# The last Y unit of each batch through DRAM, and another order of work at the tile border

## What is computed

```python
kv  = einsum('bhsd,bhse->bhde', k, v)               # 8 batches, 8 heads, 576 rows, 64 wide
y   = einsum('bhsd,bhde->bhse', q, kv)
y   = y / sqrt(mean(y*y, axis=-1) + 1e-6) * g_norm   # attention output, heads side by side: x
u   = x + ((x^T @ U) @ V)^T                          # rank 32 along the sequence
x2  = u + relu(u @ w_ch1) @ w_ch2                    # 512 -> 2048 -> 512
```

## Time and profile before

| | us |
|---|---|
| median of 3 runs (1273.92 to 1274.13) | 1274.0 |
| the profiled execution | 1274.38 |
| its span | 1272.6 |
| TensorE busy | 1250.0 (98%) |
| VectorE busy | 848.3 (67%) |
| ScalarE busy | 541.1 (43%) |
| GpSimd busy | 103.7 (8%) |

### The profile page before, as it was taken

The page is one execution under the profiler, slowest core; times in us unless marked ns, Lnnn a source line. Parts: engine busy times, 40 slices in busy tenths (PEclk is TensorE's granted clock), DMA queues, the critical chain, the costliest instruction groups (busy, mean ns, idle before and its releaser), DMA issues.

```text
span 1272.6 us, 21543 instructions
## 1 busy us (share of the span) xinstructions
PE 1250.0 (98%) x8248; PEld 1209.0 (95%) x8248; DVE 848.3 (67%) x1227; ACT 541.1 (43%) x859; POOL 103.7 (8%) x108
## 2 busy tenths in 40 slices
PE   7899999999999999999999999999999999999998
PEld 6899999999999999999999999999899898998997
DVE  5886566666656678988898988976543644445344
ACT  4664455554555446554544544543322312223120
POOL 5230000000000000000000000012202102022000
PEclk9999999999999999999999999999999999999999
DMA  9777777778677577473453628272323142240221
GB/s 210 206 188 191 184 189 209 204 188 203 175 208 194 164 246 272 136 252 132 166 177 119 239 91 275 90 202 39 102 65 84 59 102 58 66 120 29 53 59 42
DMA packets 342823, 190.46 MB, mean 150 GB/s; under 512 B 242752, under 2 KB 313296, under 8 KB 342752
## 3 DMA queue, kind: packets, MB, share of 16 engines
q1 hardware_dynamic: 338592, 184.36, 51.3%
q0 software_dynamic: 1600, 4.56, 1.4%
q10 hardware_dynamic: 2560, 0.59, 0.2%
HBM read 115.08 MB, written 72.29 MB: 147 GB/s over the span
## 4 chain that ended last, share of the span: by engine, by line
PE 91%; DVE 4%; issue 2%; DMA 2%; POOL 1%; ACT 1%; ACTq 0%; POOLq 0%; DVEq 0%
PE ps L1532 27%; PE ps L1534 27%; PE ps L1533 27%; PE ps L1553 2%; PE ps L1564 2%; PE ps L1572 1%; DMA w_raw<-in_moe_w_ch 1%; PE ps L1537 1%; DVE x_lo L1160 1%; POOL w_raw L708 1%; PE ps L1820 1%; PE ps L1823 1%; PE ps L1566 0%; PE ps L1590 0%; DVE y_hl L1096 0%
## 5 line engine op out<-in xcount | busy, mean ns | idle before, releaser
L1532 PE MATMUL ps<-x_hi,w 128*128 128x288 f32 x896 | 267.6, 299 | 3.2 <-DVE x_lo L1160 2.5
L1533 PE MATMUL ps<-x_lo,w 128*128 128x288 f32 x896 | 264.3, 295 | 0.0
L1534 PE MATMUL ps<-x_hi,w 128*128 128x288 f32 x896 | 264.0, 295 | 0.0
L1532 PE MATMUL ps<-r_hi,w_hi 128*128 128x384 f32 x672 | 224.8, 334 | 1.0 <-DVE r_lo L1320 1.0
L1533 PE MATMUL ps<-r_lo,w_hi 128*128 128x384 f32 x672 | 224.5, 334 | 0.0
L1534 PE MATMUL ps<-r_hi,w_lo 128*128 128x384 f32 x672 | 224.5, 334 | 0.0
L954 ACT ACTIVATE r_hi<-hb 128x768 fp32r<-128x768 f32 x168 | 142.5, 850 | 166.4 <-PE ps L1534 161.1
L1532 PEld LDWEIGHTS ps<-x_hi,w 128*128 128x128 f32 x896 | 168.1, 188 | 4.8 <-DVE x_lo L1160 3.3
L1534 PEld LDWEIGHTS ps<-x_hi,w 128*128 128x128 f32 x896 | 168.6, 188 | 0.0
L1533 PEld LDWEIGHTS ps<-x_lo,w 128*128 128x128 f32 x896 | 168.4, 188 | 0.0
L1322 DVE TENSOR_TENSOR r_lo<-hb,r_hi 128x768 fp32r<-128x768 f32 x120 | 114.8, 958 | 32.3 <-ACT r_hi L954 32.3
(11 more groups left out here) (168 smaller groups left out, 2332.0 us busy)
## 6 DMA issues: line engine op xcount, KB each, us to landing
hT_scratch<-h_st SPq DMA_DIRECT2D x64, 576.0 KB, 4.2
hb<-hT_scratch SPq DMA_DIRECT2D x24, 1536.0 KB, 7.2
uT_scratch<-x_raw SPq DMA_DIRECT2D x32, 288.0 KB, 3.9
x_st<-uT_scratch SPq DMA_DIRECT2D x24, 384.0 KB, 3.5
x2T_scratch<-x_st SPq DMA_DIRECT2D x24, 384.0 KB, 5.7
x_raw<-x2T_scratch SPq DMA_DIRECT2D x8, 1152.0 KB, 5.7
xt_in<-x2T_scratch SPq DMA_DIRECT2D x144, 64.0 KB, 2.5
k_raw<-in_k SPq DMA_DIRECT2D x64, 128.0 KB, 3.9
```

Source lines behind the costliest of these rows:

```text
L1532: mm(dst, ws[0], xs[0], start=first, stop=False, skip_group_check=chained)
L1533: mm(dst, ws[0], xs[1], start=False, stop=False, skip_group_check=chained)
L1534: return mm(dst, ws[1], xs[0], start=False, stop=last, skip_group_check=chained)
```

## The change

`Y_UNITS` becomes all units from 6 on, so the last unit of each batch (7, 11, up to 31) goes through DRAM too. At the tile border:

- VectorE: sums 2 and 6 and the low half of operand 1 move from steps 52 to 54 to the end of step 55, behind the transposition and addition of the last unit. Sum 4 moves from step 55 to step 1 of the next tile, behind the row sums. The low halves of operands 3 and 4 move from steps 1 and 2 to steps 2 and 4, behind the normalisation and behind the low half of Y. The q transposition of the first unit moves from row 3 to row 6 in every tile (before: in the first tile alone).
- ScalarE: the high half of operand 2 moves from step 53 into the attention copy at step 55, between its two copies. The high halves of operands 3, 4 and 5 move from steps 1, 2, 3 to 2, 3, 4.

```diff
-Y_UNITS = tuple(m for m in range(HP + 2, UNITS) if m % HP < HP - 1)
+Y_UNITS = tuple(range(HP + 2, UNITS))
...
-            def attn_copy(m, bx, by, y=y, units=0):
+            def attn_copy(m, bx, by, y=y, units=0, tile=None):
...
                 nc.scalar.activation(y[:, 0:JM, :].rearrange("p j m -> p (j m)"), ps[:, bx], ACT.Copy).then_inc(s_o, 1)
+                if tile:
+                    x_high(tile[0], tile[1], 2)
                 act.wait_ge(s_out, 2 * m + 2)
...
-            X_HIGH_AT = (27, 34, 53)
-            X_HIGH_THEN = (1, 2, 3, 6)
+            X_HIGH_AT = (27, 34)
+            X_HIGH_THEN = (2, 3, 4, 6)
...
                     elif at_ == ATT and m + 1 < UNITS:
-                        attention_evacuated(m + 1)
+                        attention_evacuated(m + 1, (t + 1, 1 - par) if r == HP - 1 else None)
+                    elif at_ == ATT:
+                        x_high(t + 1, 1 - par, 2)
...
-            X_LOW_THEN = (0, 1, 2, 5, 10)
+            X_LOW_THEN = (0, 2, 4, 5, 10)
...
                     if at_ == 1:
                         sums(m, sq)
+                        if k == 1 and not first:
+                            x_sum(t, par, 4)
...
-                    elif at_ == (6 if first and r == 0 else 3) and m + 1 < UNITS:
+                    elif at_ == (3 if r else 6) and m + 1 < UNITS:
                         q_transposed(m + 1)
...
-                    if k in (33, 53):
-                        x_low(t + 1, 1 - par, (33, 53).index(k))
-                    if k in (52, 54, 55):
-                        x_sum(t + 1, 1 - par, {52: 2, 54: 6, 55: 4}[k])
+                    if k == 33:
+                        x_low(t + 1, 1 - par, 0)
+                    if k == STEPS - 1:
+                        x_sum(t + 1, 1 - par, 2)
+                        x_low(t + 1, 1 - par, 1)
+                        x_sum(t + 1, 1 - par, 6)
...
+                    if k == 1:
+                        x_sum(t, 1, 4)
                     if k in X_LOW_THEN:
                         x_low(t, 1, 2 + X_LOW_THEN.index(k))
```

More of the change, by code:

```diff
@@ L780, in attn_copy, with attention_evacuated @@
                 nc.scalar.activation(y[:, JM, :], bank(by, 0, P), ACT.Copy).then_inc(s_o, 1)
-            def attention_evacuated(m):
-                attn_copy(m, BX, BY, units=min(m + 2, UNITS))
+            def attention_evacuated(m, tile=None):
+                attn_copy(m, BX, BY, units=min(m + 2, UNITS), tile=tile)
                 squares(m, sq)
```

## The result

| | before | after |
|---|---|---|
| median, us | 1273.96 (1273.59 to 1274.13) | 1282.88 (1281.21 to 1283.70) |
| ratio | | 1.0069, 95% interval 1.0051 to 1.0086 |
| profiled execution | 1274.38 | 1282.71 |
| its span | 1272.6 | 1280.9 |

What follows compares the result with a forecast made beforehand. The prediction took TensorE's matmuls to set the pace. Six borders (6.0 us) and the last (1.6) added 7.6 us to the profiled 1274.38: 1282.0, less 0.4 for the median, rounded to 1282; range 1274 to 1287 us.

Steps and rivals of the forecast that it cites:

- The transposes: TensorE, last unit of each batch: five transposes of Y go, 0.55 us saved for each of seven units, 3.9 in all.
- The line behind the arrival: VectorE at the border, from Y's transposition to low half 6: step 12 starts at 173.85 instead of 172.94, +0.9 us.
- break-even: Border: if Y's blocks come back at 159.1 us, freed matmuls pay for the stalls; a tie, 1275 us, chance 0.12.
- full gain: Border: with blocks there by 158.0 us TensorE never waits, each border gives 1.07 us back; 1267 us, chance 0.10.
- The stalls: TensorE at the border waits for late operands, 2.0 us in all, against 1.1 us of gain.
- The arrival: Border: Y's blocks return through DRAM, their transposition on VectorE starting 10.0 us after the normalisation's start, plus 0.1.
- The third rival: Y's DRAM trip by the fit alone: blocks back within some 6 us, kernel faster; counted in the second rival, chance 0.10.
- The moves: Border, VectorE and ScalarE: the later q transposition costs nothing; sum 4's 0.67 us is counted in the VectorE line.
- At most 0.5 us a tile: First unit's q transposition at row 6: upper cost where VectorE's idle 1.6 us no longer covers the later blocks.
- The last border: Behind unit 31: step 6 is 0.3 us late and loads of the second weight add 1.3, together +1.6 us.
- knock-on: Fourth rival: late blocks delay following units, or u's store lands late; 0.5 to 1.4 us a tile more, chance 0.08.
- The sum: Whole kernel: six borders at 0.9 + 0.1 us, 6.0 us, and 1.6 us for the last, +7.6 us.

## Why the prediction was right, step by step

**The transposes.** 0.55 us per unit expected, 0.54 found (a stretch of 14.82 or 14.83 became 14.28), and the low-rank matmuls have no wait. Right.

**The line behind the arrival.** Counted from the transposition, low half 1 was to end 3.1 us later, low half 3 7.5 and low half 6 13.8. The rows of L1164 above give 3.09 (its end at 165.10), 7.48 (169.49) and 13.72 (175.73). Added up from pitches of the earlier trace rows, start to start, it held to a tenth of a microsecond, though VectorE had never run in this order. The break-even was put at 159.1, which is D = 9.1 behind 149.96, and the borders say 9.11; the full gain at 158.0, D = 8.0, and the borders say 7.94.

**The stalls.** Steps 2, 4, 6 and 12 were named and are late. Step 8 and the low-rank part, named too, were not; TensorE had lost time at three steps by then, which is likely why.

**The arrival** is the term that was mis-sized. 10.0 us was taken, with 0.1 added at the end from the queue; 10.49 was measured, and at one to one behind D that is 0.35 us a border, 2.1 us in all. I had put twelve units in one median, and they were of two kinds. The K load stands ahead of Y's store in all of them. In the second units of a batch it is still being issued when Y is finished: the store leaves 1.2 to 1.4 us behind the start of the normalisation, and the trip has a mean of 10.37. In the third it is through by then: the store leaves at 0.86, and the trip has 9.60. The last unit of a batch is of the first kind and a little worse: its store leaves at 1.23 to 2.14, mean 1.53. From the second units alone I would have come within 0.12 us.

**What the trip is made of.** In the mean of the six borders: the normalisation 0.83 us, 0.70 until the store of Y leaves (K's loads stand ahead of it on SP), 3.1 in the middle until a store has landed, 1.3 more until the first block load leaves (V's and q's loads stand ahead), 2.3 for the four block issues, 2.2 until the transposition: 10.5. The Trainium skill, "DMA: Bandwidth & Descriptors", section "Anatomy of one DMA — SWDGE (gpsimd) path", would have a store and a load back within some 6 us of the finished Y (an estimate from its 2.0 us and 436 GB/s, for the other issuing path); the traces have 9.7. Transfer by transfer they don't contradict it: the store lands 3.1 us after its issue in the middle, a block load 2.5. What the estimate has no term for is the 0.7, the 1.3 and the four issues one behind another. The third rival was that sum, and it falls.

**The moves.** Put at nothing, they changed a border by -0.2 us where Y comes early and by +0.1 where it comes late. "At most 0.5 us a tile" for the q transposition was kept: 0.42 in one of six. The run at row 11 showed what lies beyond: five rows later, 26 us.

**The last border.** +1.6 expected, 1.12 found: the step behind the weight's additions starts at 480.55 where before had 470.98, 9.57 us later, and 8.45 of these were there at the last attention (444.75 against 436.30), ahead of unit 31. The loads of the weight came 1.1 us later against VectorE's list (4.57 instead of 3.47) where 1.9 had been counted with. The 0.55 of unit 31's freed transposes, which fall between the last attention and the tile's start, are already off the 1.12.

**What was given back.** From 480.55 on the changed kernel makes up 1.2 us: the rest of the up tile loses 0.35 more, and the down product takes 1.5 us less (349.6 against 351.1, from its first product to its last). Two waits for the low half of its operand (1.0 us in the list before) are not in the list after. The same shows in all nine kernels here in which the last units are no longer transposed on TensorE (349.6 to 350.2 us, against 350.9 to 351.3 in the other three), also where unit 31 is as before. I did not expect it, and its cause stays open.

**The sum and the luck in it.** 8.3 at six borders, 1.1 at the last, 0.4 knock-on, -0.2 in the first tile, -1.2 behind it: 8.4, and the spans differ by 8.3 us. The forecast had 7.6, from 6.0 and 1.6. The sign and the mechanism are as predicted, but that the totals lie only 0.7 apart is partly luck: the borders cost 2.3 us more than forecast, and the last border (0.5) and the down product took most of that off again.

## What to carry to other kernels

A round trip through DRAM is its landings and what is issued ahead of and between them: here some 5.3 us of two landings, 4.3 of issues and queue, and 0.8 of the operation that makes the data. Price it from units of the trace that have the same queue ahead of them, not from all that look alike, and name what its landing gates: the engine's line behind it, summed from start to start, gives a break-even before anything is built. Here 0.54 us of freed matmuls stood against a landing that every later operand of the tile waits for, and the bottleneck's own gain was the smaller number.
When a step is moved on one engine, look at which buffer it frees and which queue waits for that: the same 0.69 us cost at most 1.5 us at row 6 and 26 us at row 11.

## What the runs showed of the hardware

- L - D was 6.33 to 6.35 us in the six borders of the changed kernel, and the same in the run with the blocks ahead of q, though D varied by 1.3 us there. The engines repeat their lists to 0.02 us; what varies from border to border is the trip.
- Each part of the trip varies: in the changed kernel's six borders Y's store leaves 1.23 to 2.14 us behind the start of the normalisation, the block loads 5.58 to 6.55. Four block loads of 72 KB each, issued in 2.06 us (3.40 at one border), are all there between 1.8 and 3.2 us behind the last issue's end in the six borders (from issue to landing, of line 388, the store of Y, and line 395, the block loads):

```profile
DMA to landing us min/median/max: 2.5/3.1/4.4
...
DMA to landing us min/median/max: 2.0/2.5/3.9
```

- SP's issues are not free: four loads of this shape keep it for 2.06 us, one of K's and V's for 0.5 to 0.8, and a single one that waits for a buffer holds up all behind it: in the run at row 11 the first unit's blocks left 12.1 us behind the start of its normalisation in the tile shown, in the changed kernel 7.0.
- A wait of 2.6 to 3.6 us of TensorE was followed, in five of six places, by some 3.4 us in which its granted clock was 0.50 to 0.69. It does not follow the wait's length alone: behind one of 2.63 us it was 0.68, behind one of 2.72 us it stayed at 1.00. Behind the changed kernel's waits of at most 0.96 us at the six steady borders it was 1.00.
